# A fused attention and mixing kernel: probabilities normalised on GpSimd ahead of their transposes, value product copied by ScalarE straight into the tokens

## The reference

```
# attention, B, H, S, D = 4, 8, 576, 64: only the 32 largest scores of a row count
scores = scale * q @ k.T
kth = partition(scores, -32)[..., -32]
attn = exp(where(scores >= kth, scores, -1e9) - max)
attn = attn / (sum(attn) + 1e-9)
x = (attn @ v)                      # to [B, S, 512], heads side by side
# gated causal convolution over the sequence, 5 taps, depthwise
gate = sigmoid(conv(x, conv_w))
x = (gate * (x @ w_val)) @ w_out
# Fourier mixing over sequence and features, real part; layer norm; 4x MLP
u = x + real(fft(fft(x, axis=1), axis=2))
un = (u - mean) / sqrt(var + 1e-6)
out = u + max(un @ w_ch1, 0) @ w_ch2
```

## Time and profile before

| | |
|---|---|
| median of three runs | 1212.93 us (1212.51 to 1215.17) |
| profiled execution: its time, its span | 1214.56 us, 1212.8 us |
| TensorE busy | 1049.4 us, 87% |
| VectorE busy | 884.3 us, 73% |
| ScalarE busy | 621.3 us, 51% |
| GpSimd busy | 406.9 us, 34% |
| mean granted TensorE clock | 0.926 |

### The profile page before, as it was taken

One profiled execution on the slowest core, in us unless ns is written; L12 is line 12 of the kernel. 1 busy time (PEld: TensorE's weight loads), 2 busy tenths in 40 slices (PEclk: granted clock), 3 DMA queues, 4 the chain that ended last, 5 costly groups with the idle time before them and its releaser, 6 DMA issues.

```text
span 1212.8 us, 19844 instructions
## 1 busy us (share of the span) xinstructions
PE 1049.4 (87%) x6608; PEld 841.9 (69%) x6608; DVE 884.3 (73%) x1898; ACT 621.3 (51%) x1253; POOL 406.9 (34%) x704
## 2 busy tenths in 40 slices
PE   3776565789798989989798989999798999998998
PEld 2554454666587878866587878775587888648887
DVE  6999999996996978696996978696996970330000
ACT  3786766644565655554565655454565653012221
POOL 2444533142443332233433332322443322133221
PEclk9886756889898999999898999999898999998999
DMA  8566455021355856321355846321365655206974
GB/s 256 163 202 203 140 187 188 11 74 35 102 209 193 282 192 198 134 75 46 111 217 192 270 178 213 123 70 45 126 226 202 226 179 204 108 1 237 351 277 162
DMA packets 81188, 200.37 MB, mean 165 GB/s; under 512 B 8384, under 2 KB 26560, under 8 KB 81088
## 3 DMA queue, kind: packets, MB, share of 16 engines
q1 hardware_dynamic: 81088, 199.11, 48.2%
HBM read 177.58 MB, written 21.50 MB: 164 GB/s over the span
## 4 chain that ended last, share of the span: by engine, by line
PE 56%; issue 14%; DVE 12%; POOL 10%; ACT 5%; DMA 1%; SPq 1%; DVEq 0%; ACTq 0%; POOLq 0%
PE p_m L567 15%; PE p_m L553 15%; PE p_m L461 14%; DVE rest L742 5%; PE p_t L434 4%; PE p_t L450 4%; PE p_s L421 4%; DVE top L748 3%; ACT prob L630 2%; POOL k_lo L876 2%; POOL bias L884 1%; POOL hid_lo L949 1%; POOL w_st L901 1%; POOL bias L885 1%; DMA u<-w_ch 1%
## 5 line engine op out<-in xcount | busy, mean ns | idle before, releaser
L748 DVE MAX8 top<-rest 128x8 f32<-128x576 f32 x432 | 304.7, 747 | 0.0
L949 POOL TENSOR_TENSOR hid_lo<-hid,hid_hi 128x256 fp32r<-128x256 f32 (+1 forms) x128 | 107.0, 836 | 325.8 <-ACT hid_hi L692 325.8
L742 DVE MATCH_REPLACE8 rest<-top,rest 128x576 f32<-128x576 f32 x288 | 211.7, 743 | 0.0
L553 PE MATMUL p_m<-un_hi,w_st 128*128 128x320 f32 (+1 forms) x1024 | 172.9, 313 | 44.6 <-POOL un_lo L940 25.3
L567 PE MATMUL p_m<-w_st,hid_hi 128*128 128x512 f32 x640 | 206.3, 404 | 0.2 <-POOL hid_lo L949 0.2
L553 PEld LDWEIGHTS p_m<-un_hi,w_st 128*128 128x128 f32 x1024 | 149.6, 198 | 55.5 <-POOL un_lo L940 26.2
L630 ACT ACTIVATE prob<-s_sb,bias 128x576 f32<-128x576 f32 x144 | 111.1, 772 | 105.0 <-POOL bias L885 104.6
L623 ACT ACTIVATE s_sb<-p_s 128x576 f32<-128x576 f32 x144 | 93.1, 646 | 136.3 <-PE p_s L421 136.2
L434 PE MATMUL p_t<-id_sb,prob 128*128 128x128 f32 x720 | 122.1, 306 | 34.4 <-ACT or_sb L652 34.0
L421 PE MATMUL p_s<-k_hi,q_st 128*128 128x512 f32 (+1 forms) x320 | 118.2, 372 | 33.2 <-POOL k_lo L876 19.5
L450 PE MATMUL p_t<-pT,v_sb 128*64 128x128 f32 (+1 forms) x1600 | 106.9, 285 | 43.5 <-ACT pT L643 23.4
(11 more groups left out here) (78 smaller groups left out, 1602.9 us busy)
## 6 DMA issues: line engine op xcount, KB each, us to landing
w_st<-w_split SPq DMA_DIRECT2D x256, 512.0 KB, 4.4
w_split<-w_st SPq DMA_DIRECT2D x32, 512.0 KB, 3.0
q_raw<-qT SPq DMA_DIRECT2D x64, 144.0 KB, 3.4
k_raw<-kT SPq DMA_DIRECT2D x64, 144.0 KB, 3.4
u<-w_ch SPq DMA_DIRECT2D x32, 256.0 KB, 3.6
v_sb<-v SPq DMA_DIRECT2D x16, 256.0 KB, 3.5
wslot<-w_val SPq DMA_DIRECT2D x4, 1024.0 KB, 5.3
wslot<-w_out SPq DMA_DIRECT2D x4, 1024.0 KB, 5.3
```

The costliest lines, as they stand in the source:

```text
L553: mm = pe.matmul(mbank(HIDDEN_BANK[g], n), w1_st[i % NB1][:, w, k, :], x[:, k, at:at + n], start=part + k == 0, stop=part + k == KC + 1)
L742: dve.match_replace(rest[tt % 2][:, :], top[tt % 4][:, 8 * n - 8:8 * n], src[:, :], LOWEST).then_inc(s_chain, 1)
L748: found = dve.max(top[tt % 4][:, 8 * n:8 * n + 8], rest[tt % 2][:, :])
L949: pool.tensor_tensor(hid_lo[i % 2][:, 0:WIDTH[g]], hid[:, 0:WIDTH[g]], hid_hi[i % 2][:, 0:WIDTH[g]].bitcast(F32), ALU.subtract).then_inc(m ...
```

## The change

1. GpSimd's `normalise` multiplies a tile's probabilities in place by `rinv`, two tiles at the end of each odd slot; `transpose_p` now waits for it. `attend` loses the two matmuls with `rinv`, `store_out` copies 128 columns and not 256, straight into `x_new`, and `scale_out` and `or_sb` are gone.
2. TRANSPOSE goes from 6 to 8 and ATTEND from 7 to 9, with four `prob` buffers and not three. The steps therefore begin two slots later.
3. In ScalarE's slot `exponent` goes from ahead of the steps to the end; in GpSimd's slot `biases` goes behind the steps.
4. In STEPS `trn 0` goes ahead of `seq 2`, and `trn 1` ahead of `proj 4`; the places of VectorE's first two row normalisations and the conv slots follow.

```diff
-STEPS += [... ("proj", 3), ("seq", 2), ("trn", 0), ("proj", 4), ("trn", 1)]
+STEPS += [... ("proj", 3), ("trn", 0), ("seq", 2), ("trn", 1), ("proj", 4)]
-NORM_AT = {("proj", 2): 0, ("seq", 2): 1, ("ch0", 1): 2, ("ch0", 4): 3, ("ch0", 7): 4}
+NORM_AT = {("proj", 1): 0, ("proj", 2): 1, ("ch0", 1): 2, ("ch0", 4): 3, ("ch0", 7): 4}
-SELECT, EXPONENT, RECIP, TRANSPOSE, ATTEND = 1, 4, 6, 6, 7
+SELECT, EXPONENT, RECIP, TRANSPOSE, ATTEND = 1, 4, 6, 8, 9
+NP = 4
...
                 def transpose_p(t):
-                    pe.wait_ge(s_exp, t + 1)
+                    pe.wait_ge(s_norm, t + 1)
...
                     if t and unit_due(t + TRANSPOSE - 1):
-                        pe.wait_ge(s_or, unit_of(t + TRANSPOSE - 1 - ATTEND) + 1)
+                        pe.wait_ge(s_x, unit_of(t + TRANSPOSE - 1 - ATTEND) + 1)
...
                 def attend(t):
                     pe.wait_ge(s_pT, min(t + ATTEND - TRANSPOSE + 1, ALL_TILES))
-                    pe.wait_ge(s_rinv, t // 2 + 1)
...
-                    for h, (tt, c0) in enumerate(src):
-                        mm = pe.matmul(p_o[D * h:D * h + D, 1, 0:n],
-                                       rinv[:, tt % 4:tt % 4 + 1].broadcast_to((P, D)),
-                                       id_sb[:, c0:c0 + n], start=True, stop=True, skip_group_check=True)
...
                 def store_out(t):
...
-                    act.activation(or_sb[n_u % 2][:, :, 0:n], p_o[:, :, 0:n], ACT.Copy).then_inc(s_or, 1)
+                    at = TAPS - 1 + P * (i // 2)
+                    act.activation(x_new[p % NX][:, at:at + n], p_o[:, 0:n], ACT.Copy).then_inc(s_x, 1)
...
# ScalarE's slot
                     if split_due(s) is not None:
                         split_high(split_due(s), 0)
                         split_high(split_due(s), 1)
-                    if due(s, EXPONENT):
-                        exponent(s - EXPONENT)
...
                     for x in plan[s][1:]:
                         step(*x)
+                    if due(s, EXPONENT):
+                        exponent(s - EXPONENT)
...
# VectorE, reciprocal
                     if t >= 4:
-                        dve.wait_ge(s_pv, unit_of(t - 4) + 1)
+                        dve.wait_ge(s_norm, t - 3)
...
# GpSimd
-                def scale_out(t):
...
+                def normalise(t):
+                    pool.wait_ge(s_rinv, t // 2 + 1)
+                    p = prob[t % NP][:, 0:S]
+                    pool.tensor_scalar(p, p, rinv[:, t % 4:t % 4 + 1], None, ALU.mult).then_inc(s_norm, 1)
...
                     if split_due(s) is not None:
                         split_low(split_due(s))
-                    if due(s, EXPONENT):
-                        biases(s - EXPONENT)
...
                     for x in plan[s][0:1]:
                         step(*x)
-                    if unit_due(s):
-                        scale_out(s - ATTEND)
                     for x in plan[s][1:]:
                         step(*x)
+                    if due(s, EXPONENT):
+                        biases(s - EXPONENT)
+                    if due(s, RECIP) and (s - RECIP) % 2:
+                        normalise(s - RECIP - 1)
+                        normalise(s - RECIP)
```

More of the change, by code:

```diff
@@ L21 @@
 NS = 6
-FILLS = 17
+FILLS = 18
 TOPK = 32
@@ L68 @@
 STEPS = [("val", j) for j in range(2 * KC)] + [("zed", m) for m in (2, 0, 1)]
-STEPS += [("seq", 0), ("proj", 0), ("proj", 1), ("seq", 1), ("proj", 2), ("proj", 3), ("seq", 2), ("trn", 0), ("proj", 4),
-          ("trn", 1)]
+STEPS += [("seq", 0), ("proj", 0), ("proj", 1), ("seq", 1), ("proj", 2), ("proj", 3), ("trn", 0), ("seq", 2), ("trn", 1),
+          ("proj", 4)]
 for f in range(FC + 1):
@@ L83 @@
 CONV_AT = {21: [(0, (0, 1))], 22: [(0, (2, 3))], 23: [(0, (4,))], 28: [(1, (0, 1))], 29: [(1, (2, 3))], 30: [(1, (4,))],
-           35: [(2, (0, 1))], 36: [(2, (2, 3))], 37: [(2, (4,))], 43: [(3, (0, 1))], 44: [(3, (2, 3, 4))]}
-TANH_AT = {24: 0, 31: 1, 38: 2, 44: 3}
+           36: [(2, (0, 1))], 37: [(2, (2, 3))], 38: [(2, (4,))], 45: [(3, (0, 1))], 46: [(3, (2, 3, 4))]}
+TANH_AT = {24: 0, 31: 1, 39: 2, 46: 3}
 def steps_by_slot():
@@ L144, in build @@
         bias = [sb(f"bias{i}", [P, 2]) for i in range(4)]
-        prob = [sb(f"prob{i}", [P, SP]) for i in range(3)]
+        prob = [sb(f"prob{i}", [P, SP]) for i in range(NP)]
         psum_row = sb("psum_row", [P, 4])
@@ L148, in build @@
         pT = [sb(f"pT{i}", [P, NCH, P]) for i in range(3)]
-        or_sb = [sb(f"or_sb{i}", [P, 2, P]) for i in range(2)]
         x_new = [sb(f"x_new{i}", [P, XW]) for i in range(NX)]
@@ L173, in build @@
         p_m = ps("p_m", [P, 4 * BANK])
-        p_o = p_t[:, BANK + P:BANK + 3 * P].rearrange("p (a n) -> p a n", a=2)
+        p_o = p_t[:, BANK + P:BANK + 2 * P]
         def mbank(n, cols=BANK):
@@ L205, in build @@
         s_pv = sem("s_pv")
-        s_or = sem("s_or")
+        s_norm = sem("s_norm")
         s_x = sem("s_x")
@@ L431, in transpose_p @@
                     if t and unit_due(t + TRANSPOSE - 1):
-                        pe.wait_ge(s_or, unit_of(t + TRANSPOSE - 1 - ATTEND) + 1)
+                        pe.wait_ge(s_x, unit_of(t + TRANSPOSE - 1 - ATTEND) + 1)
                     for c in range(NCH):
-                        mm = pe.transpose(p_t[:, c * P:c * P + P], prob[t % 3][:, c * P:c * P + P], id_sb[:, :])
+                        mm = pe.transpose(p_t[:, c * P:c * P + P], prob[t % NP][:, c * P:c * P + P], id_sb[:, :])
                     mm.then_inc(s_tr, 1)
@@ L627, in exponent @@
                     act.wait_ge(s_bias, 2 * (t + 1))
-                    if t >= 3:
-                        act.wait_ge(s_tr, t - 2)
-                    act.activation(prob[t % 3][:, 0:S], s_sb[t % NS][:, :], ACT.Prelu,
+                    if t >= NP:
+                        act.wait_ge(s_tr, t - NP + 1)
+                    act.activation(prob[t % NP][:, 0:S], s_sb[t % NS][:, :], ACT.Prelu,
                                    bias=bias[t % 4][:, 1:2], scale=-BIG, alpha=1.0 / BIG).then_inc(s_drop, 1)
@@ L634, in exponent @@
                     act.wait_ge(s_drop, t + 1)
-                    act.activation(prob[t % 3][:, 0:S], prob[t % 3][:, 0:S], ACT.Exp,
+                    act.activation(prob[t % NP][:, 0:S], prob[t % NP][:, 0:S], ACT.Exp,
                                    bias=bias[t % 4][:, 0:1], scale=-SCALE,
@@ L649, in store_out @@
                     act.wait_ge(s_pv, n_u + 1)
-                    if n_u >= 2:
-                        act.wait_ge(s_x, n_u - 1)
-                    act.activation(or_sb[n_u % 2][:, :, 0:n], p_o[:, :, 0:n], ACT.Copy).then_inc(s_or, 1)
+                    p, i = tile_of(t)
+                    if p >= NX:
+                        act.wait_ge(m_gv, upto_gv((p - NX) // PAIRS + 1, 0))
+                    at = TAPS - 1 + P * (i // 2)
+                    act.activation(x_new[p % NX][:, at:at + n], p_o[:, 0:n], ACT.Copy).then_inc(s_x, 1)
                 def split_weights(i):
@@ L842, in step @@
                         normalise(b, NORM_AT[what, n])
-                for i in range(3):
+                for i in range(NP):
                     dve.memset(prob[i][:, S:SP], 0.0).then_inc(s_zero, 1)
@@ L885, in biases @@
                     pool.tensor_scalar(bias[t % 4][:, 0:1], kth, most, SCALE, ALU.subtract, ALU.mult).then_inc(s_bias, 1)
-                def scale_out(t):
-                    n_u = unit_end(t)
-                    p, i = tile_of(t)
-                    n = REST if i == TILES - 1 else P
-                    pool.wait_ge(s_or, n_u + 1)
-                    if p >= NX:
-                        pool.wait_ge(m_gv, upto_gv((p - NX) // PAIRS + 1, 0))
-                    src, x = or_sb[n_u % 2], x_new[p % NX]
-                    at = TAPS - 1 + P * (i // 2)
-                    pool.tensor_tensor(x[:, at:at + n], src[:, 0, 0:n], src[:, 1, 0:n], ALU.mult).then_inc(s_x, 1)
+                def normalise(t):
+                    pool.wait_ge(s_rinv, t // 2 + 1)
+                    p = prob[t % NP][:, 0:S]
+                    pool.tensor_scalar(p, p, rinv[:, t % 4:t % 4 + 1], None, ALU.mult).then_inc(s_norm, 1)
                 def split_weights(i):
```

4 lines of the change are left out of this document (2 added, 2 removed).

## The result

The changed kernel takes **1412.34 us** (1410.23 to 1413.31, 4 runs) beside 1213.55 us (1212.51 to 1215.17) for the kernel before: ratio 1.163 [1.161, 1.166], 199 us slower. The forecast was 1267 with a range to 1298: the sign holds, the size does not.

What follows compares the result with a forecast made beforehand. The prediction took VectorE to bound the fill and TensorE the rest: per period 24.7 us go and 41.9 come, net +17.2, +49 over three periods, +6 once only, giving 1267 us, range 1205 to 1298.

Steps and rivals of the forecast that it cites:

- The `un_lo` wait: TensorE's 7.2 us wait per period for `un_lo` shrinks as two row blocks are transposed earlier: gain 6.1 us.
- The attend term: Attend waits for `pT` of the tile transposed in the same slot: 9.9 us added per period.
- The last batch: With no tiles beside it, its `un_lo` wait drops from 3.65 to 1.1 us and a slow stretch goes: -4.5 us.
- the size of normalise: One GpSimd normalise of 128x576, on which TensorE's transposes wait, was taken to last 0.9 us.
- ring: Value stage: VectorE's gv, GpSimd's fold, bias and normalise, TensorE's next value product and gv close a loop: 2.8 us per period.
- The fill: The stretch before the steps start, two slots longer plus contention with normalise: 9 to 12 us more.
- the head behind `seq 2` and `trn 1`: Start of that TensorE slot, waiting for `un_lo`, bias, normalise and ScalarE's two copies: 3.8 us per period.
- The slow clock: Slower matmuls after stalls: 4.3 us per period gained behind old stalls, 1.5 lost behind the new 4 us ones.
- the `rinv` product: TensorE's product of `rinv` with the identity goes away, 0.32 us each, 16 or 17 times: gain 5.4 us per period.
- the three split slots: GpSimd's 3.4 us of splitting still stand ahead of `hid_lo`: 3.5 us added per period in three slots.
- The rival of the port: VectorE with two SBUF inputs and GpSimd exclude one another for whole instructions: about 1300 us, chance 0.08.
- Rival 1: TensorE doesn't wait at the slot heads, so the change is faster: about 1160 us, chance 0.12.

Runs made afterwards that it cites:

- e5: e1 with the transposes and attend one slot later, five `prob` buffers, and the steps and last conv slots moved with them: 1198.41 us.
- e4: The kernel before with only the new order of the steps and of VectorE's row normalisations: 1194.26 us.
- e1: The changed kernel with GpSimd's two biases back at the head of its slot, ahead of the steps: 1306.01 us.
- e3: The changed kernel with biases back at the head of GpSimd's slot and a normalise of one column only: 1221.64 us.
- e6: The changed kernel with eight `top` buffers in place of four: 1413.55 us.
- e10c: e9c with eight `top` buffers in place of four: 1277.03 us.
- e7: e4 with the exponential last in ScalarE's slot, old lags, biases at the head, no normalise on GpSimd: 1171.36 us.
- e11c: e1 with both normalises at the head of GpSimd's slot, behind the biases and ahead of the steps: 1190.18 us.
- e2: The changed kernel with a normalise of one column in place of 576: 1323.94 us.
- e9c: The changed kernel, biases last, with the transposes and attend one slot later, five `prob` buffers and e5's conv slots: 1292.14 us.
- e8: e1 with the normalise on ScalarE, as a Copy with a scale behind `pT` in odd slots: 1197.32 us.

## Why the prediction was right in sign and wrong in size

**Right: where TensorE would wait.** "transpose_p(s-8) stands at the head of TensorE's slot and waits for a normalise" is what the profile shows: TensorE's largest wait, all 176.9 us of it in even slots, and 15.5 left where e5 gives it slack. The `un_lo` wait is gone, with 21 us gained in e4 beside it. The attend term (9.9) measured 9.4 in the period, and slot by slot too: 2.90 in slot 55 (3.2), 2.20 each in 59 and 61 (2.4), 1.43 in 53 and 57 together (1.9). The last batch (-4.5) came out at -6.7. What the text named as a sign of a wrong size, "if normalise takes 0.3 or 1.5, the size is off", came true upwards.

**Wrong, first: the size of normalise, 0.9 us.** It measures 1.75, outside the bounds 0.30 and 1.40. "The length is paid for, and the second input with it" fails: this one-input instruction takes longer than the two-input one of the same size (L876, 1.40 alone). It is not a meeting with VectorE either that makes it long: the shortest of the 144 takes 1.72 and the median 1.75.

```profile
L887 POOL TENSOR_SCALAR prob<-prob,rinv x144: 1724/1748/2322, 46.8 to 1219.9; 128x576 f32<-128x576 f32 x144
```

From the 769 ns for 512 elements in the Trainium skill ("GPSIMD Engine Reference", the elementwise accounting) the prediction had worked out an estimate of 0.87, and the trace disagrees by a factor of two.

The prediction's own slope was 4.2 us of kernel for each 0.1 of normalise (25 for 0.6); e1 and e3 give 84 us for 1782 less 328 ns, 5.8 for each 0.1. By the forecast's slope 0.85 us more make +35, and 1267 becomes 1302. e1, the kernel with the biases where the sum had them, measured 1306. The agreement is in good part luck: with the thin normalise the same sum says 1242 and e3 measured 1222, so the other terms were some 20 too high where the slope was too low.

**Wrong, second, and larger: the place of the biases.** "GpSimd's order around the slot change (steps, then bias) was however already the one that counts here, so its lateness can be read directly." The order of GpSimd's own queue is indeed nearly the old one. But the lateness was read from a kernel in which the exponential of that bias stood after the scores copy and `pT` of its slot; now it stands ahead of the next slot's. So the old lateness does not carry over: a bias's delay comes back through scores copy, `pT`, relu and `hid_lo` into the next bias (4.95 us in the timeline above). The prediction found the order "bias, exponential, scores copy, `pT`" for attend, but did not follow it on to `hid_lo` and round to the next bias; its "ring" was the value stage's alone, at 2.8, and there the heads wait 10.4. Cost of the biases' place: 106 us (e1). It also did not read `select`, where VectorE waits for the bias of four tiles ago; that proved worth nothing in the changed kernel (e6) and 15 us once the rest is loosened (e10c).

Together, by measurement: with both undone e3 is 6.5 us above the kernel before, where the sum had 28; the length of the normalise is worth 84 (the sum had 25 between 0.3 and 0.9 us); the place of the biases is worth 106 (the sum had nothing). That is 197 of the 199 measured, against 53 forecast. It is close because the shares were measured one behind the other; it does not confirm the single terms.

**The fill** was forecast at +12 (two slots and contention) and is +57.4. Of it 24.6 is the biases (e1), and 8.1 the length of the normalise once they are back (e1 against e3). e3 still has +24.7, 13 more than forecast; e7, without the two slots, has +2.6. e11c, with the two slots, a full normalise and no work ahead of it but splits and biases, has +13.1, and VectorE is busy 13.0 us longer in it: that is the forecast of 12 for the slots. The slots are therefore priced rightly, and what the prediction missed of the fill is again the heads. It had them wait only where TensorE bounds, but in the fill of the changed kernel the transposes wait 40.7 us as well.

**A slip in the sum:** the terms of the head behind `seq 2` and `trn 1` add up to 3.4, not 3.8; the trace has 3.8, which is chance.

**The slow clock** was forecast at 1.5 a period behind the new stalls, less 4.3 behind the old ones. TensorE's busy time grew by 7.0 a period instead, although the `rinv` product went out of it.

**Terms not tested apart:** the three split slots and the `rinv` product (5.4 per period). For the product there is a bound: TensorE is busy 245.1 us in e7's period, which has it, and 243.9 in e11c's, which has not, at granted clocks of 0.98 and 0.97. Scaled to one clock that is an estimate of 4 us at most.

**The rivals.** The rival of the port does not stand as the cause: a MAX8 takes 751 ns in the changed kernel and 746 before, the normalise itself is hardly ever stretched (median 1748, shortest 1724), and the two-input subtraction k_lo takes 1960 ns on GpSimd with the full normalise and 1956 with the thin one (e2), so its mean's rise from 1597 before is not due to the normalise's length. Rival 1 (TensorE doesn't wait at the heads) is what e5 and e11c build by other means: 1198 and 1190, not its 1160.

**Open.** Of the biases' cost without slack, how much goes over the head of TensorE's slot and how much over ScalarE: e9c shows 94 us over ScalarE and VectorE with the head relaxed, e1 106 with it tight, and the two are not additive shares. No run has the biases last and the exponential in its old place, so that the ring needs both is read from the timeline and not shown by a run. The 13 us of e3's fill are absent in e11c, so they seem to hang on the normalise's place behind GpSimd's steps, but no run takes that apart, and e3's profile is of its longest execution. Why e5, e8 and e11c are each faster than I expected is not shown either. That e8 gains as much as e5 may lie in the shorter instruction or in its place; e11c says that the place is enough, not that the length does nothing.

## What to carry to other kernels

Work moved to the tail of one engine's slot and awaited at the head of another's can cost what it lasts in every slot where the waiting engine has nothing to spare, however idle its own engine is (84 us for 1.45 us more of normalise, e1 and e3); the same work at the head of the slot, or one slot of skew more, took 116 or 108 us less (e11c, e5). Two instructions moved last in their slots can close a ring over two slots (bias, exponential, copies, relu, `hid_lo`, bias), though one of them moved alone is a gain (e7; the other was not tried alone): follow a late result once round until it comes back to its own engine before reading its lateness from the old trace. And a change of four parts should be tried in parts: the order of the steps and the place of the exponential gave 3.5% (e7), where the whole lost 16%.
